# A fused FFT filter and two gated dense layers on one core: tile rows put 2048 bytes apart, and the first loads reordered

## The reference

```python
X = np.fft.rfft(x, axis=1)
y = np.fft.irfft(X * (filt_r + 1j * filt_i)[None], n=3008, axis=1)
t = y.reshape(6016, 256)
h = t @ moe_w_in                      # 256 -> 2048
t = np.where(h > 0, h, exp(min(h, 0)) - 1) @ moe_w_out
h = t @ moe2_w_in
out = (h * clip(h + 3, 0, 6) / 6) @ moe2_w_out
```

## Time and profile before

| | |
|---|---|
| median of 3 runs | 1099.59 us (1098.49 to 1100.38) |
| the profiled execution | 1099.54 us, of which the span of its instructions is 1097.7 us |
| TensorE busy | 1092.4 us (100% of the span), 4798 matmul instructions |
| weight loads | 882.6 us (80%) |
| VectorE, ScalarE, GpSimd busy | 767.5, 755.0, 295.2 us (70%, 69%, 27%) |
| DMA | 77.24 MB, mean 70 GB/s |

### The profile page before, as it was taken

One profiled execution on the slowest core, in us unless ns is written; L12 is line 12 of the kernel. 1 busy time (PEld: TensorE's weight loads), 2 busy tenths in 40 slices (PEclk: granted clock), 3 DMA queues, 4 the chain that ended last, 5 costly groups with the idle time before them and its releaser, 6 DMA issues.

```text
span 1097.7 us, 13426 instructions
## 1 busy us (share of the span) xinstructions
PE 1092.4 (100%) x4798; PEld 882.6 (80%) x4798; DVE 767.5 (70%) x940; ACT 755.0 (69%) x1141; POOL 295.2 (27%) x233
## 2 busy tenths in 40 slices
PE   9999999999999999999999999999999999999998
PEld 4667888888888888888888888888888888888887
DVE  7998666767777777777676666665665665666665
ACT  0555788797797797787888566566666666666654
POOL 5658211514514514514120220120121021020000
PEclk9999999999999999999999999999999999999999
DMA  9754200302302302302244301001101101100001
GB/s 309 222 173 172 95 1 28 140 1 79 141 1 87 132 1 89 131 1 90 91 159 154 132 1 38 38 1 38 38 1 38 39 1 37 39 1 1 38 1 38
DMA packets 33811, 77.24 MB, mean 70 GB/s; under 512 B 3664, under 2 KB 20048, under 8 KB 33744
## 3 DMA queue, kind: packets, MB, share of 16 engines
q1 hardware_dynamic: 27984, 67.03, 17.6%
q10 hardware_dynamic: 5760, 9.35, 2.5%
HBM read 46.35 MB, written 30.02 MB: 70 GB/s over the span
## 4 chain that ended last, share of the span: by engine, by line
PE 99%; DVE 0%; ACT 0%; issue 0%; ACTq 0%
PE ps L501 47%; PE ps L490 14%; PE ps L492 14%; PE ps L491 14%; PE ps L453 3%; PE ps L421 3%; PE ps L429 2%; PE ps L438 1%; PE ps L440 1%; PE ps L441 1%; PE ps L459 0%; DVE g_lo L822 0%; ACT g_hi L707 0%; PE ps L524 0%; PE ps L522 0%; PE ps L520 0%
## 5 line engine op out<-in xcount | busy, mean ns | idle before, releaser
L822 DVE TENSOR_TENSOR g_lo<-e,g_hi 128x502 fp32r<-128x502 f32 (+1 forms) x288 | 295.6, 1054 | 135.6 <-ACT g_hi L707 135.6
L490 PE MATMUL ps<-op_hi,w_hi 128*128 128x502 f32 (+1 forms) x672 | 262.5, 391 | 0.0
L492 PE MATMUL ps<-op_lo,w_hi 128*128 128x502 f32 (+1 forms) x672 | 261.9, 390 | 0.0
L491 PE MATMUL ps<-op_hi,w_lo 128*128 128x502 f32 (+1 forms) x672 | 261.2, 389 | 0.0
L501 PE MATMUL ps<-g_lo,w_hi 128*128 128x502 f32 (+1 forms) x764 | 235.6, 389 | 0.1
L501 PE MATMUL ps<-g_hi,w_hi 128*128 128x502 f32 (+1 forms) x764 | 234.7, 388 | 0.0
L501 PE MATMUL ps<-g_hi,w_lo 128*128 128x502 f32 (+1 forms) x764 | 234.3, 387 | 0.0
L916 POOL TENSOR_TENSOR op_lo<-op_raw,op_hi 128x1004 fp32r<-128x1004 f32 (+3 forms) x48 | 100.4, 2091 | 455.3 <-ACT op_hi L644 455.3
L501 PEld LDWEIGHTS ps<-g_lo,w_hi 128*128 128x128 f32 x764 | 142.9, 188 | 30.3 <-DVE g_lo L822 2.0
L501 PEld LDWEIGHTS ps<-g_hi,w_lo 128*128 128x128 f32 x764 | 143.7, 188 | 29.1
L501 PEld LDWEIGHTS ps<-g_hi,w_hi 128*128 128x128 f32 x764 | 143.5, 188 | 28.8
(11 more groups left out here) (82 smaller groups left out, 1153.3 us busy)
## 6 DMA issues: line engine op xcount, KB each, us to landing
w_parts<-w_out SPq DMA_DIRECT2D x16, 704.0 KB, 3.1
op_raw<-y SPq DMA_DIRECT2D x30, 251.0 KB, 3.7
x_ring<-x_dev SPq DMA_DIRECT2D x32, 192.0 KB, 4.9
w_hi<-w_parts SPq DMA_DIRECT2D x8, 704.0 KB, 4.0
w_lo<-w_parts SPq DMA_DIRECT2D x8, 704.0 KB, 5.4
y<-ystage SPq DMA_DIRECT2D x10, 502.0 KB, 3.1
out_dev<-ystage SPq DMA_DIRECT2D x10, 502.0 KB, 3.1
y<-ystage ACTq DMA_DIRECT2D x18, 235.0 KB, 2.7
```

The lines of the kernel that those rows point to most:

```text
L490: pe.matmul(out, w_hi[p][:, cols], hi, start=start, stop=False, skip_group_check=True)
L491: pe.matmul(out, w_lo[p][:, cols], hi, start=False, stop=False, skip_group_check=True)
L492: pe.matmul(out, w_hi[p][:, cols], lo, start=False, stop=True, skip_group_check=True).then_inc(done, 1)
L822: return dve.tensor_tensor(g_lo[:, tiles, :], e[:, tiles, :], f32(g_hi[:, tiles, :]), ALU.subtract)
```

## The change

Rows of `op_hi`, `op_raw`, `op_lo`, `g_hi`, `g_lo`, `e` and `h2` get a pitch of 512 float32, of which 502 are used as before; the spacer grows from 16 to 48 float32, and `h2` and `e` change places. Input 0 is loaded from ScalarE's queue, ahead of the signs; SP begins with A, input 1, BX, input 2. In SP's loop the input comes before the filter, and the filter is that of step i + 3 instead of i + 4. The weights of the first layer are loaded and rounded at other steps: `w_step(p)` = 8 + 5p // 2 (8, 10, 13, 15, 18, 20, 23), loads three steps ahead. The third warm-up matmul has 256 columns instead of 512.

```diff
--- before.py
+++ after.py
@@ -38,6 +38,8 @@
 
 
 T = 502
+ROW = 512
+SPACE = 48
 NS = -(-TOK // (2 * T))
 LAST_T = (TOK - (NS - 1) * 2 * T) // 2
 PAIRS = F // (2 * P)
@@ -140,13 +142,13 @@
         w_raw = sbuf(ctx, "w_raw", [P, 2, 12 * P])
         with ExitStack() as early:
             f_kept = sbuf(early, "f_kept", [P, GROUPS, 2, XCOL])
-        op_hi = [sbuf(ctx, "op0_hi", [P, 7, T], F32R)]
+        op_hi = [sbuf(ctx, "op0_hi", [P, 7, ROW], F32R)]
         with ExitStack() as raw:
-            op_raw = [sbuf(raw, "op0_raw", [P, 7, T])]
-        op_lo = [sbuf(ctx, "op0_lo", [P, 7, T], F32R)]
+            op_raw = [sbuf(raw, "op0_raw", [P, 7, ROW])]
+        op_lo = [sbuf(ctx, "op0_lo", [P, 7, ROW], F32R)]
         b12 = sbuf(ctx, "b12", [P, T])
         ystage = sbuf(ctx, "ystage", [P, 2, 2 * T])
-        sbuf(ctx, "spacer", [P, 16])
+        sbuf(ctx, "spacer", [P, SPACE])
         with ExitStack() as fft:
             mats = sbuf(fft, "mats", [P, len(MATS) * P])
             sign = sbuf(fft, "sign", [P, K2])
@@ -156,15 +158,17 @@
             prod_r = sbuf(fft, "prod_r", [P, 2, XCOL])
             prod_i = sbuf(fft, "prod_i", [P, 2, XCOL])
             back = sbuf(fft, "back", [P, 2, J, P])
-        op_hi.append(sbuf(ctx, "op1_hi", [P, 7, T], F32R))
+        op_hi.append(sbuf(ctx, "op1_hi", [P, 7, ROW], F32R))
         with ExitStack() as raw:
-            op_raw.append(sbuf(raw, "op1_raw", [P, 7, T]))
-        op_lo.append(sbuf(ctx, "op1_lo", [P, 7, T], F32R))
-        g_hi = sbuf(ctx, "g_hi", [P, 4, T], F32R)
-        g_lo = sbuf(ctx, "g_lo", [P, 4, T], F32R)
-        e = sbuf(ctx, "e", [P, 4, T])
-        h2 = sbuf(ctx, "h2", [P, 2, T])
+            op_raw.append(sbuf(raw, "op1_raw", [P, 7, ROW]))
+        op_lo.append(sbuf(ctx, "op1_lo", [P, 7, ROW], F32R))
+        g_hi = sbuf(ctx, "g_hi", [P, 4, ROW], F32R)
+        g_lo = sbuf(ctx, "g_lo", [P, 4, ROW], F32R)
+        h2 = sbuf(ctx, "h2", [P, 2, ROW])
+        e = sbuf(ctx, "e", [P, 4, ROW])
         w_out = sbuf(ctx, "w_out", [P, 2, WCOL], F32R)
+        op_hi, op_raw, op_lo = ([t[:, :, 0:T] for t in group] for group in (op_hi, op_raw, op_lo))
+        g_hi, g_lo, e, h2 = (t[:, :, 0:T] for t in (g_hi, g_lo, e, h2))
         ps = ctx.enter_context(nc.psum_tensor("ps", [P, 8, 512], F32))
 
         def f32(ap):
@@ -288,7 +292,7 @@
                 eng.wait_ge(y_stored[t], 16 * s)
 
         def load_step(p):
-            return p + 1 if p < 2 else w_step(p) - 3
+            return w_step(p) - 3
 
         def width(s):
 
@@ -299,7 +303,7 @@
             return (2 * s - 2, 2 * s - 1) if 1 <= s <= PAIRS // 2 else ()
 
         def w_step(p):
-            return 5 + 3 * p
+            return 8 + 5 * p // 2
 
         block = ctx.enter_context(nc.Block())
 
@@ -358,9 +362,8 @@
                              ystage[:, t].rearrange("p (o t) -> p o t", o=2)[:, :, 0:n]).then_inc(y_stored[t], 16)
 
             sp.dma_start(mat("A"), mats_dev[:, 0:P]).then_inc(mat_loaded["A"], 16)
-            load_x(0)
+            load_x(1)
             sp.dma_start(mat("BX"), mats_dev[:, P:2 * P]).then_inc(mat_loaded["BX"], 16)
-            load_x(1)
             load_x(2)
             sp.dma_start(mats[:, 2 * P:], mats_dev[:, 2 * P:]).then_inc(mat_loaded["back"], 16)
             load_f(1)
@@ -369,10 +372,10 @@
             load_x(4)
             load_f(3)
             for i in range(NG):
-                if i + FSLOTS - 1 < NG:
-                    load_f(i + FSLOTS - 1)
                 if i and i + XSLOTS - 1 < NG:
                     load_x(i + XSLOTS - 1)
+                if i and i + FSLOTS - 2 < NG:
+                    load_f(i + FSLOTS - 2)
                 if i == FIRST_OP - 2:
                     sp.wait_ge(prod_ready, 3 * GROUPS)
                     load_xr(0)
@@ -455,9 +458,9 @@
                 last.then_inc(i_done, 1)
 
             pe.wait_ge(zeroed, 1)
-            for _ in range(3):
-                pe.matmul(ps[:, 0, :], back[:, 0, 0, :], back[:, 0, 0:4, :].rearrange("p j d -> p (j d)"),
-                          start=True, stop=True)
+            for cols in (4, 4, 2):
+                pe.matmul(ps[:, 0, 0:cols * P], back[:, 0, 0, :],
+                          back[:, 0, 0:cols, :].rearrange("p j d -> p (j d)"), start=True, stop=True)
             pe.wait_ge(mat_loaded["A"], 16)
             part_a(0)
             part_a(1)
@@ -675,6 +678,7 @@
                 else:
                     act.activation(dst, src, ACT.Relu, bias=3.0).then_inc(ready, 1)
 
+            act.dma_start(x_ring[0:AROWS, 0], x_dev[ORDER[0]][:, 0:GCOL]).then_inc(x_loaded[0], 16)
             act.dma_start(sign[:], sign_dev).then_inc(sign_loaded, 16)
             act.dma_start(f_kept[:, 0].rearrange("p a n -> p (a n)"),
                           f_dev[ORDER[0] // B, :, 0]).then_inc(f_kept_loaded[0], 16)
```

## The result

The kernel after the change takes **1090.65 us** (median of 6 runs, 1088.76 to 1092.32), the one before 1099.42 beside it (6 runs); the ratio is 0.9918, 95% interval [0.9908, 0.9928]. The forecast was 1096.0. So the sign is right and the size is not: -8.8 us, where the forecast said -3.5 (its terms -3.7). The profiled execution took 1091.74 us, its span is 1089.9 us, 7.8 less than the 1097.7 of before.

The account below looks back on a forecast made before the run. The prediction took TensorE's pace through its own queue to bound the kernel. 1099.54 - 3.3 (aligned rows) - 0.4 (start) + 0 (loads) = 1095.8, rounded to 1096 us; own range 1093 to 1099, 8 in 10 1072 to 1109.

Parts of the forecast that it names:

- Part 1: Aligned rows, TensorE's matmuls: 0.226 us each, 10.17 us a unit of 45 instead of 10.20, -3.3 us.
- the fast bound: Fast end for the aligned rows: 0.223 us a matmul, 10.05 us a unit, -14 us.
- rival (a): A common place locks TensorE's pace low, every matmul at 0.223 us: 1085 us, at lowest 1073; chance 0.25.
- The quick six: Quickest six matmuls in the even unit of the earlier trace, read as 1.34 us, 0.223 us a matmul.
- Rival (c): Moving rows sharing the weights' place slow matmuls: 1105 us at 0.228 us each, +29 us at 0.233; chance 0.23.
- Rival (b): The rows' place has no effect of weight, a unit stays at 10.20 us: 1099 us; chance 0.12.
- Rival (d): TensorE's excess over streaming goes altogether, 0.212 us a matmul, a price in the sixties; chance 0.02.
- Part 2: Shorter warm-up and earlier first input: TensorE starts 0.85 us sooner, worth -0.4 us, bounds -0.9 and +0.5.
- Part 3: Fourier stage, order and time of filter and weight loads: 0 us, bounds 0 and +2.
- It fits, by 0.6 us: Weight rounding two steps apart: sums ready at 40.1 us, ScalarE comes to that rounding at 40.65.
- the range for 8 in 10: Wide range for the kernel's time: 1072 to 1109 us.

Follow-up runs that it names:

- e1: Kernel before the change with the aligned rows alone, start, order of loads and weight steps as before: 1089.15 us, ratio 0.9908.
- e3: Kernel after the change with its rows packed as before (2008 bytes apart, spacer of 16): 1100.05 us, ratio 1.0011.
- p2: Kernel after the change with all tiles behind `w_raw`, so all moving rows, moved by 256 bytes: 1098.12 us, one run.
- p3: Kernel after the change with high and low halves 256 bytes apart, so place changes within each product: 1091.02 us, one run.
- p1: Kernel after the change with every moving row beginning 32 bytes later in its 512: 1104.72 us, one run.
- r3: Kernel after the change with all tiles behind `w_raw` moved by 64 bytes: 1102.66 us, one run.
- r2: Kernel after the change with the old start (input 0 on SP's queue, three full warm-up matmuls): 1090.23 us, ratio 0.9928.
- e4: Kernel before the change with aligned rows and the new start, filter order and weights as before: 1092.67 us, ratio 0.9942.
- e2: Kernel after the change with the first layer's weights requested and rounded at the steps of before: 1090.04 us, ratio 0.9915.
- q1: Kernel after the change with tiles of 504 columns and 488 for the last slice: 1094.52 us, one run.

## Why the prediction was right and wrong

**That TensorE's pace bounds the kernel, and that the place of the rows moves it.** Right. The whole gain comes with the rows (e1 -10.0, e3 +0.9 us), and no wait was taken away. Place alone doesn't fix the pace: p2 has two at one place.

**Part 1, the size.** This is the step that failed: "After the change none changes place, so I take 0.226 for all". The measured pace is 223.3 ns, the fast bound (0.223) and rival (a), which I had at 0.25. Three things were wrong in it. I took the change of place between neighbours for the cause, and p3 shows that a change by 256 bytes costs nothing while p1 shows that one common place can be slow. And I argued that quick pieces don't last over six matmuls, so that a mean over pieces is the best guess; but with aligned rows the distances settle in a short sequence that lasts for hundreds of us. And the sum was loose: 5.43 / 24 is 0.2263, which gives 10.18 us a unit and -2.3 us, where rounding to 0.226 gave -3.3. That the fast bound came out to the digit is luck. The quick six of the earlier trace rows weren't a sample of the new pace: by the starts in nanoseconds they go 222, 229, 227, 228, 223, 221, in all 1.350 us or 225.0 ns a matmul, and only the chain's pieces, cut at modelled ends, made it 1.34. The 498-column steps were put in with the rest; they went the other way (+1.1 us). With 10.05 for 80 units and 10.20 for 16 the term would have been -11.3 us, and the waits, allowed to move by 4 us, moved by 0.9.

**Rival (c)**, a shared place with the weights as a cost, falls: the rows at the weights' place run at the quick pace, and after its wait p2, at another, runs at the same 10.05. But its price, 0.233 us a matmul, exists, as the second pace of p2. **Rival (b)** falls with e1 and e3, and with p1 and r3, by 0.15 to 0.21 us a unit between places (one execution each). The Trainium skill ("SBUF — State Buffer", section "Who interferes with whom") says that TensorE waits on no other engine in this memory, and that section names no place at which rows should start. The traces don't show whether it waits for another engine there; that place matters, they do: the same rows at 32, 64 and 0 bytes gave 1104.72, 1102.66 and 1090.65 us. **Rival (d)** falls too. The Trainium skill ("TensorE: Matmul & The Clock Gate", section "Back-to-back issue gap") gives N / 2.4 + 2.5 ns for an isolated matmul, an estimated 215.8 ns for 512 columns, 211.7 for 502 and 210.0 for 498; the runs have 226.7, 223.3 or 233.3, and 226.7, so no one gap fits them.

**Part 2, the start.** The first input matmul at 5.9 us was right within what executions of one start differ by: with the short warm-up it came at 5.38 to 5.88 in ten profiles, with the full one at 6.21, 6.73, 6.73 and 6.73. Within each set the difference is the moment at which the distance of the warm-up passes halves, not the input. What failed is that -0.4 us would reach the end. No gain is seen at the end: r2, without it, takes no longer, and by itself (e4) the start costs 3.5 us. The rows had the warning, DMA engines busy for 0.71 of the Fourier stage: TensorE that starts sooner there asks for its inputs sooner, and e4 shows it waiting for them, 5.0 us in all.

**Part 3, loads and weights.** "It fits, by 0.6 us" failed. I had reckoned the sums ready at 40.1 us from GpSimd's own work, with no term for the landing of the load that they read. Moved three steps ahead of the rounding, it was issued at 29.54 and landed at 40.53, so the sums were ready at 42.4. The wait of ScalarE is 3.8 us in all (predicted as possible, at up to 2 us on the path), the gap of TensorE 1.1 + 0.3, in four of the eight profiles with these steps. Against the weights' old steps that is no loss: e2 has its gap of 0.9 at another place. The filters a step later were costed at nothing; under the new start they are a gain of about 2.6 us (e4 to e2).

**Left out.** ScalarE, VectorE and GpSimd on aligned rows were costed at nothing "because TensorE waited 3.8 us for them in 988". In the dense layers that held. At the Fourier stage's end, where GpSimd (busy 17 of the last 21 us) is on the path, it didn't: two sums 0.2 us longer each, and a gap of 0.77 us in e1 that wasn't there before.

The forecast's own range, 1093 to 1099, missed 1090.65; the range for 8 in 10, which reached to rival (a), holds it. Rival (a)'s sum had -14.8 us where the spans have -7.8. The distance of 7.0 us is the 498-column steps (16 x 0.15 = 2.4 us over 10.05), a mean of 10.20 taken for units that took 10.19 on the average (0.7), dense layers that start 2.5 us later where 0.4 sooner was forecast (2.9), the waits (0.9) and the tail (0.25), to 0.2 us.

**Open.** What rule ties pace, columns and place together, and which of the two paces an execution falls into. Places 0, 32, 64 and 256 bytes and six widths are too few to say, and the weights' place and the PSUM side weren't varied. Common shifts of under 32 bytes weren't tried, and p1, p2, p3, q1 and r3 are single executions.

## What to carry to other kernels

Where TensorE is busy all the time, measure the distance of starts of back-to-back matmuls for each width and each place of the moving rows: here 512 columns cost as much as 498 (226.7 ns), and 32 bytes of shift cost 4.7 ns a matmul in the one execution that was taken. Choose tile width and pitch by that table and not by proportion: the widest tile on whole pitches of 2048 bytes gave the best kernel (1085.10 us). Where the last slice gets fewer columns, narrow the other engines' instructions with it: here they kept their full width, and TensorE waited for them. Cost a load that is requested later with its landing under the DMA traffic of its new place, and a sooner start with the waits for inputs behind it: here it gained nothing or cost 3.5 us.

## What the hardware showed that was not expected

- The same code with the same places ran at 10.50 us a unit for its first 19 units and then, behind a wait of 0.4 us, at 10.05 for the rest (p2; the steps of 498 columns at 10.20). If the wait did it, it made every later unit of 502 columns 0.45 us quicker; one case.
- The mean distance of starts is no smooth function of columns: 488 columns 220.0 ns, 498 226.7, 502 223.3 (or 233.3), 504 226.7, 512 226.7, 448 202.7. The distances repeat after 1 matmul (488, 504, 512 columns, and the slow pace of 502), 3 (498), 4 (502) or 5 (448: 199, 206 or 207, 203, 202, 203 ns). One round always takes a whole multiple of 6.67 ns to 0.1 ns: 220.0 is 33, 226.7 is 34, 233.3 is 35, 680.0 is 102, 893.3 is 134 and 1013.4 is 152 of them. The places off 0 fit too: p1's round of 5 is 1140.0 (171), those of r3, of 4, are 906.7 and 920.1 (136 and 138). The packed rows have no such round.
- Rows 32 bytes off: 228.0 ns with 502 columns, unchanged 226.7 with 498. Rows 64 bytes off: 226.7 with 502, 230.0 with 498. Rows 256 bytes off: as at 0 behind the wait, 233.3 with 502 columns before it.
- The warm-up's clock level (1.2 GHz, passes 0.85 us apart) gave way to the upper one (2.4 GHz, passes of 512 columns 0.43 us apart) at different times in executions whose TensorE had done the same until then: with the same full warm-up, between the starts of the fifth and the sixth pass in e1 (5.03 and 5.78 us, first input at 6.21), and only behind the sixth in the kernel before (6.73).
